# A fused attention and gated feed-forward kernel: the attention front of one batch element moved together, and the orders of three engines changed with it

## The reference

```python
p_packed = sm_attn(p, k, v)                  # softmax(p k^T / 8) v: 32 rows per head
out = sm_attn(q, p_packed, p_packed)         # softmax over 32 columns
x = out as (8, 576, 512)
gate = sigmoid(sum_k conv_w[k] * x[s - 4 + k])     # 5 taps, causal
x = (gate * (x @ w_val)) @ w_out
h = relu(x @ w_in)                           # 1024 wide
u, v = h[..., :512], h[..., 512:]
v_n = layer_norm(v)
v_s = w_spatial @ v_n + b_spatial            # over the positions
result = (u * v_s) @ moe2_w_out
```

## Time and profile before

| | |
|---|---|
| median of 3 runs | 618.58 us (615.94 to 619.18) |
| profiled execution, time | 620.26 us |
| profiled execution, span | 618.5 us |
| TensorE busy | 568.5 us (92%) |
| VectorE busy | 456.2 us (74%) |
| ScalarE busy | 308.5 us (50%) |
| HBM read, written | 35.42 MB, 9.44 MB |
| mean granted TensorE clock | 0.974 of full speed |

### The profile page before, as it was taken

One profiled execution on the slowest core, in us unless ns is written; L12 is line 12 of the kernel. 1 busy time (PEld: TensorE's weight loads), 2 busy tenths in 40 slices (PEclk: granted clock), 3 DMA queues, 4 the chain that ended last, 5 costly groups with the idle time before them and its releaser, 6 DMA issues.

```text
span 618.5 us, 11858 instructions
## 1 busy us (share of the span) xinstructions
PE 568.5 (92%) x4734; PEld 385.5 (62%) x4734; DVE 456.2 (74%) x855; ACT 308.5 (50%) x481; POOL 10.3 (2%) x16
## 2 busy tenths in 40 slices
PE   4878886999989999799989999799989999899997
PEld 2335445676667757576557757576557757575785
DVE  2469699995698839895698839895698838895540
ACT  3247528376346545466345545466345545473412
POOL 0000000000000000000000000000000000000000
PEclk9979898899999999999989999999989999899999
DMA  8930640004400152004400062004400110002001
GB/s 284 325 131 2 234 156 0 2 1 158 155 0 2 39 195 76 0 0 157 153 0 0 38 195 77 0 0 157 153 0 0 38 38 0 0 0 77 0 2 76
DMA packets 24037, 45.13 MB, mean 73 GB/s; under 512 B 1937, under 2 KB 11153, under 8 KB 22994
## 3 DMA queue, kind: packets, MB, share of 16 engines
q1 hardware_dynamic: 19410, 35.42, 17.2%
q10 hardware_dynamic: 4608, 9.44, 4.1%
HBM read 35.42 MB, written 9.44 MB: 73 GB/s over the span
## 4 chain that ended last, share of the span: by engine, by line
issue 73%; PE 21%; DVE 4%; ACT 1%; POOL 0%; POOLq 0%; ACTq 0%; DVEq 0%
PE X L453 7%; PE X L469 5%; PE X L414 3%; PE X L431 2%; PE Y L395 2%; DVE vn L762 1%; DVE vn_l L610 1%; PE Y L381 1%; PE Y L318 0%; DVE prob L680 0%; DVE pack_max L639 0%; ACT u_res L992 0%; DVE prob2T_f L686 0%; PE Y L287 0%; POOL rstd L275 0%
## 5 line engine op out<-in xcount | busy, mean ns | idle before, releaser
L702 DVE SCALAR_TENSOR_TENSOR gate<-xT,conv_sb,gate 128x576 f32<-128x576 f32 x128 | 95.2, 813 | 12.5 <-ACT gate L992 12.5
L453 PE MATMUL X<-wsp_h,vn_h 128*128 128x288 f16 x320 | 67.4, 293 | 16.4 <-DVE vn_h L610 16.4
L741 DVE BATCH_NORM_STATS2 bn<-vn 128x6 f32<-128x512 f32 (+1 forms) x40 | 27.5, 690 | 72.5 <-ACT vn L1055 71.5
L431 PE MATMUL X<-gvT_h,wfused_h 128*128 128x288 f16 x256 | 54.2, 295 | 6.4 <-ACT u_res L1075 6.4
L1055 ACT ACTIVATE vn<-X,undo_v 128x512 f32<-128x512 f32 x32 | 22.0, 687 | 68.1 <-PE X L414 68.1
L453 PE MATMUL X<-wsp_h,vn_l 128*128 128x288 f16 x256 | 54.3, 295 | 0.0
L453 PE MATMUL X<-wsp_l,vn_h 128*128 128x288 f16 x256 | 53.9, 293 | 0.0
L431 PE MATMUL X<-gvT_l,wfused_h 128*128 128x288 f16 x256 | 53.9, 293 | 0.0
L431 PE MATMUL X<-gvT_h,wfused_l 128*128 128x288 f16 x256 | 53.7, 292 | 0.0
L469 PE MATMUL X<-gatedT_h,wfin_h 128*128 128x288 f16 x256 | 52.3, 286 | 0.3 <-DVE gatedT_l L611 0.3
L469 PE MATMUL X<-gatedT_l,wfin_h 128*128 128x288 f16 x256 | 52.3, 286 | 0.0
(11 more groups left out here) (159 smaller groups left out, 1121.1 us busy)
## 6 DMA issues: line engine op xcount, KB each, us to landing
k_sb<-kT SPq DMA_DIRECT2D x16, 576.0 KB, 5.1
q_sb<-qT SPq DMA_DIRECT2D x8, 1152.0 KB, 5.1
outT<-u_res ACTq DMA_DIRECT2D x32, 288.0 KB, 2.1
v_sb<-v_rows SPq DMA_DIRECT2D x8, 1024.0 KB, 5.2
stage_b<-w_in SPq DMA_DIRECT2D x2, 1024.0 KB, 14.7
stage_b<-w_spT SPq DMA_DIRECT2D x1, 1152.0 KB
v_sb<-v_rows SPq DMA_DIRECT2D x8, 128.0 KB, 5.3
stage_a<-w_outT SPq DMA_DIRECT2D x1, 1024.0 KB, 10.3
```

The source lines that it names most:

```text
L431: last = mm(X[1 - c % 2][:, a, 0:HALF], w[:, e, c * P:(c + 1) * P], x[:, e, a * HALF:(a + 1) * HALF], start=e == 0 and i == 0, stop=e == C ...
L453: last = mm(X[1 - c % 2][:, a, 0:HALF], x, w[:, a * HALF:(a + 1) * HALF], start=i == 0, stop=i == len(terms) - 1)
L702: tap = nc.vector.scalar_tensor_tensor(gate[:, j, :], xT[:, j, k:k + S], conv_sb[:, j, k:k + 1], gate[:, j, :], ALU.mult, ALU.add)
L741: nc.vector.bn_stats(bn6[0:rows, t, :], vn[0:rows, t, :]).then_inc(stats_ready, 1)
```

## The change

On TensorE, `packed_product` follows directly on the transposes, with `v_tile` 1 behind it; `packed_transpose` and `scores2` stand next to each other before `v_tile` 2, and `packed_value` before `v_tile` 3; `packed_sums` comes before the u chunks; `value` 2 comes before `final` 0. `spatial` asks for the low halves of its first chunk one tile at a time, no longer for all five. The fused v product runs over the slices m of the contraction in the outer loop, on four banks at once. VectorE and ScalarE get new orders, some of their helpers are cut in two so that the parts can stand apart, and on SyncE the prologue loads k, v, q first and then the weights in eight parts with a semaphore for each pair.

```diff
-            sp.dma_start(woutT_sb[:, :, :], w_outT.rearrange("(c p) n -> p c n", p=P)).then_inc(w_loaded, 16)
+            load_q(0, first=True)
+            w_out_rows = w_outT.rearrange("(c p) n -> p c n", p=P)
             w_in_rows = w_in.rearrange("(c p) n -> p c n", p=P)
-            sp.dma_start(win_sb[:, :, D:2 * D], w_in_rows[:, :, D:2 * D]).then_inc(w_loaded, 16)
-            load_q(0, first=True)
+            for m in range(CH):
+                sp.dma_start(woutT_sb[:, m, :], w_out_rows[:, m, :]).then_inc(w_loaded[m], 16)
+                sp.dma_start(win_sb[:, m, D:2 * D], w_in_rows[:, m, D:2 * D]).then_inc(w_loaded[m], 16)
...
@@ spatial
-                    pe.wait_ge(vn_split, ST * b + ST)
...
                 for i, (x, w) in enumerate(terms):
+                    if c == 0 and i % 3 == 0:
+                        pe.wait_ge(vn_split, ST * b + i // 3 + 1)
...
@@ fused product
+            def fuse_v(m):
+                pe.wait_ge(w_loaded[m], 32)
+                for e in range(CH):
+                    last = mm(X[e // 2][:, e % 2, 0:D], woutT_sb[:, m, e * P:(e + 1) * P], win_sb[:, m, D:2 * D],
+                              start=m == 0, stop=m == CH - 1)
+                    if m == CH - 1:
+                        last.then_inc(fuse_done, 1)
...
@@ TensorE, prologue
-            fuse(0, 0)
             packed_transpose(0)
             scores2(0)
-            fuse(0, 1)
+            fuse_v(0)
+            fuse_v(1)
             packed_value(0, first=True)
-            fuse(0, 2)
+            fuse_v(2)
             packed_sums(0)
-            fuse(0, 3)
+            fuse_v(3)
             attention_out(0, 0, first=True)
-            fuse(1, 0)
+            fuse_u(0)
             attention_out(0, 1)
+            value(0, 0)
+            fuse_u(1)
+            value(0, 1)
+            fuse_u(2)
             fuse_sums(0)
...
@@ TensorE, iteration
                 transposes1(n, 1)
-                v_tile(b, 1)
                 packed_product(n, 0)
                 packed_product(n, 1)
+                v_tile(b, 1)
+                packed_transpose(n)
+                scores2(n)
                 v_tile(b, 2)
-                packed_transpose(n)
+                packed_value(n)
+                if first:
+                    late_sums()
                 if first:
                     pe.wait_ge(fuse_gain, 2)
                 v_tile(b, 3)
-                scores2(n)
                 v_tile(b, 4)
-                packed_value(n)
-                if first:
-                    late_sums()
+                packed_sums(n)
+                if first:
                     pe.wait_ge(fuse_split, 2)
                 u_chunk(b, 0)
                 u_chunk(b, 1)
                 u_chunk(b, 2)
-                if first:
-                    pe.wait_ge(late_gain, 1)
-                packed_sums(n)
                 u_chunk(b, 3)
                 spatial(b, 0, first)
...
                 value(n, 1)
+                value(n, 2)
                 final(b, 0, first)
                 final(b, 1)
-                value(n, 2)
...
```

More of the change, by code:

```diff
@@ L169, in build_program @@
         consts_ready = sem("consts_ready")
-        w_loaded = sem("w_loaded")
+        w_loaded = [sem(f"w_loaded{m}") for m in range(CH)]
         win_u_loaded = sem("win_u_loaded")
@@ L681, in softmax2_scale, with prob2_turn @@
                                         ALU.mult).then_inc(prob2_ready, 1)
-            def prob2_turn(n):
+            def prob2_turn(n, i):
+                u = UNIT_ORDER[i]
                 dve.wait_ge(prob2_ready, n + 1)
-                for u in UNIT_ORDER:
-                    nc.vector.transpose(prob2T_f[:, u, :], prob2[:, u, :]).then_inc(prob2_turned, 1)
+                nc.vector.transpose(prob2T_f[:, u, :], prob2[:, u, :]).then_inc(prob2_turned, 1)
             def prob2_low(n, i):
@@ L873, in _ @@
             pack_pairs(0)
-            softmax2_sub(0, 0)
+            softmax2_turn(0)
+            softmax2_max(0, 0)
+            softmax2_sub(0)
             softmax2_sums(0, 0)
             softmax2_scale(0, 0)
-            prob2_turn(0)
-            pack_magnitudes(0)
+            prob2_turn(0, 0)
+            prob2_turn(0, 1)
+            packed_magnitudes(0)
+            value_magnitudes(0)
             pack_gains(0, 0)
@@ L882, in _ @@
             prob2_low(0, 1)
-            for e in range(CH):
-                fused_magnitude(0, e)
+            fused_magnitude(0, 0)
+            fused_magnitude(0, 1)
             convolve(0, 0, 0)
+            fused_magnitude(0, 2)
+            fused_magnitude(0, 3)
+            convolve(0, 2, 0)
             fused_gain(0)
-            convolve(0, 2, 0)
             gate_value(0, 0)
@@ L909, in iteration @@
                     fused_gain(1)
-                else:
-                    stats(b, 0)
-                stats(b, 1)
+                stats(b, 0)
                 pack(n, 0, base)
@@ L926, in iteration @@
                     undo_u_gain(0, base)
-                stats(b, 4)
                 variance(b, base)
-                softmax2_sums(n, base)
+                softmax2_scale(n, base)
                 norm(b)
-                pack_magnitudes(n)
-                softmax2_scale(n, base)
-                prob2_turn(n)
-                for t in range(ST):
-                    vn_low(b, t)
+                prob2_turn(n, 0)
+                u_magnitude(b, 0)
+                u_magnitude(b, 1)
+                vn_low(b, 0)
+                vn_low(b, 1)
+                vn_low(b, 2)
+                u_magnitude(b, 2)
+                vn_low(b, 3)
+                vn_low(b, 4)
                 if first:
                     late_low_spatial()
-                for c in range(CH):
-                    u_magnitude(b, c)
-                pack_gains(n, base)
+                u_magnitude(b, 3)
                 prob2_low(n, 0)
+                pack_low(n)
+                gated_gains(b, base)
+                prob2_turn(n, 1)
+                gated(b, 0)
                 prob2_low(n, 1)
-                gated_gains(b, base)
-                pack_low(n)
-                gated(b, 0)
                 gated(b, 1)
@@ L950, in iteration @@
                 gated(b, 2)
+                gate_value(n, 0)
                 gated(b, 3)
@@ L1122, in _ @@
             read_transposes1(0, 1)
-            read_fused(0, 0)
             read_packedT(0)
             softmax2_exp(0)
-            read_fused(0, 1)
-            for u in range(UNITS):
-                read_packed_value(0, u)
-            high_prob2(0, 0)
-            read_fused(0, 2)
-            high_packed(0)
-            read_fused(0, 3)
-            high_prob2(0, 1)
+            read_packed_values(0)
+            high_prob2(0, 0)
+            high_packed(0)
+            high_prob2(0, 1)
+            read_fused(0, 0)
+            read_fused(0, 1)
             act.wait_ge(conv_loaded, 16)
@@ L1161, in iteration @@
                     high_fused(1)
-                else:
-                    relu_v(b, 0)
                 read_transposes1(n, 0)
                 read_transposes1(n, 1)
+                if not first:
+                    relu_v(b, 0)
+                read_packedT(n)
                 relu_v(b, 1)
                 relu_v(b, 2)
-                read_packedT(n)
+                read_packed_values(n)
+                softmax2_exp(n)
                 relu_v(b, 3)
                 relu_v(b, 4)
-                for u in range(UNITS):
-                    read_packed_value(n, u)
-                softmax2_exp(n)
                 relu_u(b, 0)
```

105 lines of the change are left out of this document (55 added, 50 removed).

## The result

The changed kernel took 601.85 us (median of 4 runs, 600.91 to 603.11) against 618.88 us for the kernel before, measured beside it (median of 4, 615.94 to 619.61). The ratio is 0.9735, interval 0.9698 to 0.9772: 2.65% faster. The forecast was 599 with a range of 593 to 609. The profiled execution took 602.28 us with a span of 600.5 us and a mean granted clock of 0.983. A second set of five runs of the same kernel gave 602.04 us.

The account below looks back on a forecast made before the run. The prediction took TensorE as the bound, with only its gaps to win. Span 618.5 + 0.4 (prologue and first iteration) - 20.3 (loop) = 598.6, then + 1.76 - 1.68 = 598.7, so 599 us; range 593 to 609.

Parts of the forecast that it names:

- The loop: Six loop turns: turns of 66.2 us as spatial's and attention_out's waits go, 397.0 us against 417.3, so -20.3 us.
- The two new waits: TensorE's front in each turn: 0.33 us before packed_product for transpose copies, 0.50 us before scores2 for the packedT copy.
- The case of one fall a turn: Loop: short gaps drop TensorE's clock once a turn, 6 x 1.0 us back, 605 us; part of a rival at 0.14.
- The prologue: Prologue: scores2 3.8 us earlier and the 3.6 us wait gone; lead 4.9, or 3.0 if the clock drops; 3.9 taken.
- The first iteration: First iteration: late weights delay u chunk 3 and spatial; 3.1 to 5.5 us longer, 4.3 taken.
- tail: Tail after the loop: keeps its order, spatial did not wait there, and its 54.24 us stay.
- The front waits and the clock: Rival, chance 0.14: front gaps at upper ends, 11 us back, 610; or a clock fall once a turn, 605.
- The lead kept: Rival, chance 0.15: the first iteration's waits are shorter than walked; 4 us more gained, 595 us.
- VectorE as the bound: Rival, chance 0.10: VectorE's loop operations come 1.5 us later, 0.9 us a turn returns, 604 us.
- Slow slices: Rival, chance 0.03: prologue weight slices land at a third of the rate, packed_value waits 5 us for wval_sb, 604 us.
- The second transpose of prob2: Rival, chance 0.04: in each turn it waits on VectorE behind gated_gains; 5 us late gives 70.3 us turns, 624 us.

Follow-up runs that it names:

- Experiment 2: The changed kernel with spatial's one wait for all five low halves put back: 612.39 us, ratio 0.9911 to the kernel before.
- experiment 4: The changed kernel with one more maximum a turn on VectorE, into a column nothing reads, before the last maximum of u: 602.79 us.
- experiment 3: The changed kernel with v_tile 2 put back between packed_transpose and scores2 in all iterations: 606.10 us.
- Experiment 8: Experiment 7 with late_gains and the undo factor of u moved right behind softmax2_sub on VectorE: 601.23 us.
- experiment 11: The changed kernel as it stands, run once more beside experiments 3, 8 and 9: 602.04 us.
- Experiment 7: The changed kernel with ScalarE's fused copy, high_fused(1), moved behind the copies of the transposes in the first iteration: 602.08 us.
- experiment 9: Experiment 8 with the first iteration rebuilt: late copies in two parts, spatial(0) waiting tile by tile, u_sums after spatial(1), other helpers reordered: 595.27 us.
- experiment 10: Experiment 9 with spatial(0) waiting once for all late halves instead of tile by tile: 599.69 us.
- experiment 5: The changed kernel with three more maxima on VectorE in every turn, 2.0 us: 611.59 us.
- experiment 6: The changed kernel with the first q load moved behind the eight weight slices: 604.69 us.

## Why the prediction came out as it did

*The loop: right.* Forecast 397.0 us, measured 396.82. Spatial was put at 32.66 us after scores1 and started at 32.74; the last low half at 34.2, measured 34.3; gated(0) and spatial(2) at 39.9 and 40.6, measured 39.8 and 40.7; the convolution from 42.95 to 48.9, measured from 42.86 for 5.92. Experiment 2 confirms the 1.5 us given to the finer wait (a wait of 1.4, a turn 1.6 longer), and experiment 4 that VectorE's slack is real.

*The two new waits: right.* Forecast 0.33 and 0.50 us a turn; the trace records 0.21 and 0.41. The ends of products are modelled in it, so a recorded idle time may be somewhat short; the front as a whole agrees with the larger numbers: packed_sums starts 236.03 - 215.29 = 20.74 us after scores1, where 20.60 was forecast. The 3 us that the prediction adds for both waits at their lower ends are 0.5 a turn; its working gives 0.28 of that for the first wait and names no lower end for the second.

*Clock in the loop.* The six turns together have a clock of 1.00. The case of one fall a turn, which would have given 605, fell. The rule of the Trainium skill that the prediction weighed against this is stated in TensorE: Matmul & The Clock Gate, in the section "A second HAM failure mode: psum-queue depth-cycling", which follows the section that the prediction names: short idle times of TensorE between groups of products made the clock of a kernel go up and down. With one fall a turn, at the 1.0 us of the earlier trace rows, the loop would have gained 14 us; the trace does not agree with the rule at 0.21 or at 0.41 us in the loop.

*The prologue: right within 0.4 us.* A lead of 3.9 was taken, between 4.9 without and 3.0 with a fall of the clock; it was 3.53 in the profiled execution. Both cases exist: scores2 took 2.17 us here, with the window from 18.70 at a clock of 0.50, and 1.20 us in the profiles of experiments 3 and 8, whose prologues end at 60.2 and 60.3. The fall costs less than the 1.9 us that it was given: from the start of scores2 to the end of the prologue it is 62.02 - 18.70 = 43.32 us with it and 60.17 - 17.74 = 42.43 without, 0.9 us. The other 1.0 us between these two profiles was there before scores2. The wait of 3.60 us for `pack_max` is gone, as forecast, and `attention_out` starts at 37.6 where 35.9 was forecast, the 1.0 us of the clock and the late start of scores2 ahead of it.

*The first iteration: the right mechanism, the size too small.* This is the term that missed. Forecast +4.3 (3.1 to 5.5), measured +5.97. Both waits were named, at L433 and for `wsp_tail`. The first was 3.3 us (forecast 3 to 4). The second was given 4.1 us and took 6.2: TensorE was ready at 108.2, 46.2 us into the stage (forecast 47.0), and the weights came at 52.4 (forecast 51.1). The 6.2 itself is in part chance, as experiment 11 shows (3.4 in a second profile); what sets the stage is when the weights come, and that was 52.4 in both. From the start of spatial to the next scores1 it then took 149.38 - 114.45 = 34.93 us against 146.94 - 112.96 = 33.98 before, and the window behind the wait has a clock of 0.58. So the 5.97 us are 5.0 of a later start of spatial (52.4 for 47.4 before) and 0.95 behind it; of the 1.7 us by which the forecast missed, 1.3 are the later weights.

The step that failed stands in the prediction as "softmax2_turn starts 21.9 us after the stage's beginning", with late_gains ending at 33.6. They were at 24.25 and 97.02 - 62.02 = 35.0. I had priced neither the fused copy of 1.99 us ahead of the copies of the transposes, which the cover v_tile 1 no longer hides, nor the low clock behind the waits of the front (5.12 us for the forty products of L320). The low clock behind the wait at spatial was in the range, at up to 2.4 us, and cost about 1. Experiment 7 shows that the first alone is not the cause: without it the turn starts at 21.90, just as forecast, and pack_gains comes at 31.4 as before. TensorE, slowed behind its longer wait, now holds it. Experiment 8 shows that the late gains alone are not it either. What removes the loss is experiment 9, all of its edits together, and experiment 10 shares it out: the wait for whole tensors is the larger part. How much each of the other edits in experiment 9 brings was not tried.

*The sum.* Terms against measurement: prologue +0.4, first iteration +1.7, loop -0.2, tail +0.1, together +1.9 us of span (598.6 forecast, 600.5 measured). The other 1.2 us of the difference between 598.7 and 601.85 come from the last step: I subtracted 1.68 us because the median of before was below its profiled execution by that much, and after the change it is only 602.28 - 601.85 = 0.43 below.

*The rivals.* The front waits and the clock: fell. The lead kept: fell for the changed kernel; it is what experiment 9 then built. VectorE as the bound: fell (experiments 4 and 5), with about 0.9 us to spare. Slow slices: fell; packed_value starts at 28.36 in the prologue with no wait, and waits 0.50 us for `wval_sb` in the profile of experiment 3, not 5. The second transpose of prob2: in the turn the convolution started 0.1 us from its forecast, so nothing was late there; delays of 4 us were not tried.

## What to carry to other kernels

A finer wait is worth only what stands behind it: alone it moved the same 2.7 us to the waits behind it, and with the producer's queue reordered it was worth 1.6 us a turn. A stage that runs once deserves the same walk as the loop, with every one-time copy on each queue in it; here almost a third of the loop's gain was given back there, and in the rebuilt stage 4.8 of 7.1 us hung on one wait for whole tensors that could be taken tile by tile. When a wait is shortened, look at the clock of the stretch behind the next one before the gain is counted. And the length of a wait is no measure of its cost while the engine's arrival varies: compare when the awaited thing comes.

## What the runs showed of the hardware

The same gaps were followed by either clock. In each profile of the changed prologue but that of experiment 6, TensorE idles 1.17 us before packed_transpose and 0.41 us before scores2. The changed kernel, and experiment 3:

```profile
17.95 0.33 PE L289 MATMUL Y<-ident,packed_pair 128*128 128x128 f32 x1 [1.17 <-DVE packed_pair L639]
18.70 2.17 PE L349 MATMUL Y<-q_sb,packedT 64*32 64x288 f32 x32 [0.41 <-issue]
```

```profile
17.74 1.20 PE L349 MATMUL Y<-q_sb,packedT 64*32 64x288 f32 x32 [0.41 <-issue]
```

The 32 products take 2.17 us in one and 1.20 in the other, and from their start the prologue takes 43.32 and 42.43 us more. In the first iteration the same program waited 3.32 us before u chunk 3 in both of its profiles; the pairs of products behind the wait took 0.42 us in one and up to 0.69 in the other (experiment 11). Why one execution falls and the other doesn't was not settled. In the loop 0.41 us at the same place never did it.

The clock can take back an earlier start whole. In experiment 7 packed_value began 2.3 us earlier in the stage, behind a wait 1.6 us longer, and the 4.63 us at the lower level that followed brought TensorE to packed_sums no earlier than in the changed kernel.
